# Expert groups of up to three tiles in one fixed pass, with the first layer computed already turned

## The reference

```python
scores = np.where(mask, scale * q @ k.T + bias, -1e9)       # window 128, batch 4, 8 heads, seq 576, dim 64
x = (softmax(scores) @ v).transpose(0, 2, 1, 3).reshape(2304, 512)
logits = x @ w_gate                                          # 8 experts
expert_idx = np.argmax(logits, axis=1)
gate_w = softmax(logits)[np.arange(N), expert_idx]
# each expert takes its tokens in order, up to capacity (576)
h = np.maximum(disp @ w1[e], 0.0)                            # [rows, 512] @ [512, 1024]
y = h @ w2[e]                                                # [rows, 1024] @ [1024, 512]
out[i] = gate_w[i] * y[expert_idx[i], pos[i]]
```

## Time and profile before

| what | value |
|---|---|
| median of 3 runs | 413.89 us (413.81 to 414.29) |
| profiled execution, its own time | 414.16 us |
| its span, first to last instruction | 412.5 us |
| mean granted TensorE clock | 0.993 |
| PE busy | 398.3 us (97%) |
| DVE, ACT, POOL busy | 254.8, 200.1, 146.0 us |

### The profile page before, as it was taken

One profiled execution on the slowest core, in us unless ns is written; L12 is line 12 of the kernel. 1 busy time (PEld: TensorE's weight loads), 2 busy tenths in 40 slices (PEclk: granted clock), 3 DMA queues, 4 the chain that ended last, 5 costly groups with the idle time before them and its releaser, 6 DMA issues.

```text
span 412.5 us, 10630 instructions
## 1 busy us (share of the span) xinstructions
PE 398.3 (97%) x2630; PEld 326.3 (79%) x2631; DVE 254.8 (62%) x802; ACT 200.1 (49%) x530; POOL 146.0 (35%) x228
## 2 busy tenths in 40 slices
PE   7999999999999999999999999999999999999991
PEld 7688888887877777888888888888888888888871
DVE  6787776889798578755566355526755566323220
ACT  2978778877867434555333155223555433122210
POOL 7548888725634423123221123221122221122201
PEclk9999999999999999999999999999999999999997
DMA  9999999999320115656766235706556760111100
GB/s 163 194 294 210 239 235 248 287 229 213 75 78 28 53 27 191 219 207 206 248 226 184 95 107 201 244 25 188 182 197 199 245 216 25 51 51 40 51 25 17
DMA packets 80971, 64.08 MB, mean 155 GB/s; under 512 B 63726, under 2 KB 63726, under 8 KB 80944
## 3 DMA queue, kind: packets, MB, share of 16 engines
q1 hardware_dynamic: 73600, 52.19, 46.4%
q0 software_dynamic: 3520, 10.76, 8.0%
q10 hardware_dynamic: 3824, 0.80, 1.2%
HBM read 54.29 MB, written 10.23 MB: 156 GB/s over the span
## 4 chain that ended last, share of the span: by engine, by line
PE 89%; DVE 4%; SPq 3%; DMA 1%; issue 1%; POOL 0%; ACT 0%; POOLq 0%; DVEq 0%
PE ps L1431 30%; PE ps L1463 18%; PE ps L1467 9%; PE ps L1264 7%; PE ps L1291 7%; PE ps L1451 4%; PE ps L1302 4%; PE ps L1236 4%; PE ps L1272 3%; PE ps L1424 2%; SPq L360 2%; DMA q_rows<-in_q 1%; DVE ps L871 1%; DVE probs L884 1%; PE ps L1348 0%
## 5 line engine op out<-in xcount | busy, mean ns | idle before, releaser
L1431 PE MATMUL ps<-weights_sb,rowsT_hi 128*128 (+1 forms) x336 | 107.8, 402 | 0.0
L809 ACT ACTIVATE hidden<-ps 128x512 f32<-128x512 f32 x20 | 12.0, 598 | 141.4 <-PE ps L1431 89.5
L1463 PE MATMUL ps<-weights_sb,hiddenT_hi 128*128 x320 | 79.2, 390 | 0.5 <-ACT hiddenT_hi L813 0.5
L1168 DVE TENSOR_TENSOR weights_sb<-raw,weights_sb 128x1024 f32 (+1 forms) x56 | 67.1, 1219 | 15.6 <-issue 13.3
L646 POOL DMA_INDIRECT out<-y_sb,dst_now x20 | 20.2, 1008 | 151.5 <-DVE y_sb L1175 151.5
L1431 PEld LDWEIGHTS ps<-weights_sb,rowsT_hi 128*128 128x128 f32 x336 | 61.1, 188 | 13.9 <-issue 0.6
L1463 PEld LDWEIGHTS ps<-weights_sb,hiddenT_hi 128*128 128x128 f32 x320 | 60.0, 188 | 13.3 <-issue 0.7
L1431 PE MATMUL ps<-weights_sb,rowsT_lo 128*128 (+1 forms) x168 | 66.2, 394 | 0.0
L1148 DVE TENSOR_TENSOR hiddenT_lo<-ps,hiddenT_hi 128x512 fp32r<-128x512 f32 x40 | 25.8, 686 | 57.2 <-ACT hiddenT_hi L813 57.2
L798 ACT ACTIVATE weights_sb<-raw 128x1024 f32 (+1 forms) x56 | 56.6, 1068 | 0.0
L696 ACT ACTIVATE probs<-probs,mins 128x128 f32<-128x128 f32 x144 | 55.6, 393 | 0.2 <-DVE mins L884 0.2
(11 more groups left out here) (177 smaller groups left out, 602.2 us busy)
## 6 DMA issues: line engine op xcount, KB each, us to landing
raw<-in_moe_w SPq DMA_DIRECT2D x64, 512.0 KB, 4.1
q_rows<-in_q SPq DMA_DIRECT2D x16, 256.0 KB, 6.0
v_rows<-in_v SPq DMA_DIRECT2D x16, 256.0 KB, 5.7
x_rows<-x_sb SPq DMA_DIRECT2D x16, 256.0 KB, 4.7
k_rows<-in_k SPq DMA_DIRECT2D x14, 256.0 KB, 5.9
k_rows<-in_k ACTq DMA_DIRECT2D x2, 256.0 KB, 7.2
v_rows<-in_v SPq DMA_DIRECT2D x4, 128.0 KB, 6.3
v_front<-in_v SPq DMA_DIRECT2D x4, 128.0 KB, 6.1
```

The costliest lines, as they stand in the source:

```text
L1168: vec.tensor_tensor(weights_sb[:, slot, 2 * layer + 1, part].rearrange("p s n -> p (s n)"), raw[:, j, :], weights_sb[:, slot, 2 * layer, p ...
L1431: ins = te.matmul(dst, left[a], right[c], start=first and n == 0, stop=last and n == 2)
L1463: te.matmul(y_ps(j), hiddenT[0][:, c, :], weights(slot, kind, D * c, D), start=(c == 0 and kind == 2), stop=False)
```

## The change

Experts are done one after another in a fixed pass, `group(n)` for n = 0 to 7, each with up to three tiles side by side (two for expert 0, whose first tile is done as before). The first layer now holds a 128x128 piece of the weights and moves the tiles' turned rows, 256 or 384 columns at once, so that the hidden layer comes out already turned; PE has no `turn_hidden`. The hidden features are made in eight chunks `c`; chunk c's second layer stands two steps behind its first, so a group has ten steps, and three PSUM banks and three SBUF buffers go round (`RINGED`). From expert 1 on, each step asks whether the expert has a third tile (`third`) and takes the code for three or for two. The three gathers, row transposes, weighings and scatters of a group are always done, also where the third tile is empty. Weight blocks are split in a fixed order, one per step, with addresses known beforehand. Tiles beyond the third of an expert go through a loop at the end, with their weights loaded again. Most of DVE's table arithmetic (`make_tables`) now stands behind the first chunk of group 0.

```diff
-    PAIRS = -(-MOST // 2)
-    TILES = 2 * PAIRS + 3
+    SIDE = 3
+    TABLE = -(-N // P)
+    RINGED = 3
+    TURNED_AT = (3, 4, 5)
...
-        hidden_ps = lambda half: ps[:, half, :]
-        hiddenT_ps = lambda half: ps[:, 2 + half, :]
-        rowsT_ps = ps[:, 4, :]
-        y_ps = lambda j: ps[:, 5 + j, :]
+        first_hidden_ps = lambda half: ps[:, half, :]
+        first_hiddenT_ps = lambda half: ps[:, 2 + half, :]
+        first_y_ps = ps[:, 5, :]
+        hiddenT_ps = lambda c, size: ps[:, c % RINGED, 0:P * size]
+        y_ps = lambda i: ps[:, RINGED + i, :]
+        rowsT_ps = lambda i: ps[:, 6 + i % 2, :]
...
+            def gather(n):
+
+                if not (isinstance(n, int) and n == 0):
+                    pool.wait_ge(rows_turned, tiles_before(n))
+                    pool.wait_ge(weight_kept, n)
+                if isinstance(n, int) and n > 0:
+                    rows = src_row[:, KEEPS * n:KEEPS * n + SIDE]
...
+                for i in range(sides(n)):
+                    wait_alone(pool, y_ready, tile_count(n, i))
+                    g.indirect_dma_start(out, bass.IndirectOffsetOnAxis(ap=rows[:, i:i + 1], axis=0),
+                                         y_sb[:, i, :], None, bounds_check=N - 1, oob_is_err=False
+                                         ).then_inc(scattered, 16)
...
+            gather(0)
             pool.wait_ge(first_y_ready, 1)
             g.indirect_dma_start(out, bass.IndirectOffsetOnAxis(ap=first_dst_i[:, 0:1], axis=0),
                                  first_y[:, :], None, bounds_check=N - 1, oob_is_err=False
                                  ).then_inc(first_scattered, 16)
-            pool.wait_ge(tables_ready, 1)
+            gather(1)
+            gather(2)
             pool.wait_ge(dst_ready, 1)
             pool.wait_ge(first_scattered, 16)
-            tiles = pool.value_load(tiles_to_i[0:1, E - 1:E], min_val=1, max_val=TILES)
-            with pool.Fori(0, PAIRS) as pair:
-                with pool.If(pair * 2 + 1 <= tiles):
-                    for o in (1, 2):
-                        t = pool.snap(pair * 2 + o)
-                        with pool.If(t < tiles):
-                            gather(t + 2, o % 2)
-                        with pool.If(t <= tiles):
-                            if o == 2:
-                                finish_scatter(t - 2)
-                            else:
-                                with pool.If(pair > 0):
-                                    finish_scatter(t - 2)
-                            scatter(t - 1, (o + 1) % 2)
-            pool.wait_ge(scattered, tiles * 16)
+            scatter(0)
+            for n in range(1, E):
+                if n + 2 < E:
+                    gather(n + 2)
+                finish_scatter(n - 1)
+                scatter(n)
...
+            def relu(n, c):
+                size = sides(n)
+                act.wait_ge(hidden_done, n * FC + c + 1)
+                nc.scalar.activation(hiddenT[0][c % RINGED][:, 0:P * size], hiddenT_ps(c, size),
+                                     ACT.Relu).then_inc(hiddenT_hi, 1)
+
+            def group(n):
+                for c in range(FC):
+                    relu(n, c)
+                    if n + 1 < E:
+                        split_hi(c // CHUNKS, n + 1, c % CHUNKS)
+                        if c in TURNED_AT:
+                            rows_hi(n + 1, c - TURNED_AT[0])
...
+            def lower(n, c):
+                size = sides(n)
+                dve.wait_ge(hiddenT_hi, n * FC + c + 1)
+                vec.scalar_tensor_tensor(out=hiddenT[1][c % RINGED][:, 0:P * size], in0=hiddenT_ps(c, size), scalar=0.0,
+                                         in1=hiddenT[0][c % RINGED][:, 0:P * size].bitcast(F32),
+                                         op0=ALU.max, op1=ALU.subtract).then_inc(hiddenT_ready, 1)
...
+            def weigh_all(n):
+                dve.wait_ge(weight_kept, n + 1)
+                if not (isinstance(n, int) and n == 0):
+                    dve.wait_ge(y_free, n)
+                for i in range(sides(n)):
+                    weigh(n, i)
+
+            def group(n):
+                for c in range(FC):
+                    lower(n, c)
+                    if n == 0 and c == 0:
+                        make_tables()
+                    if n + 1 < E:
+                        split_lo(c // CHUNKS, n + 1, c % CHUNKS)
+                        if c in TURNED_AT:
+                            rows_lo(n + 1, c - TURNED_AT[0])
+                        if c == TURNED_AT[-1]:
+                            keep_weights(n + 1)
+                weigh_all(n)
+
+            for i in range(SIDE - 1):
+                rows_lo(0, i)
+            keep_weights(0)
...
+            def make_tables():
+                link(vec.scalar_tensor_tensor(out=is_free[:, :], in0=is_free[:, :], scalar=float(2 * N),
+                                              in1=src_f[:, :], op0=ALU.mult, op1=ALU.add))
+                vec.tensor_copy(dst_row[:, :], is_free[:, :]).then_inc(dst_ready, 1)
+                te = [P, TABLE, E]
+                vec.tensor_scalar(extra[:, 1:E], tiles_of[:, 1:E], -float(SIDE), 0.0, ALU.add, ALU.max)
...
+            for n in range(E):
+                group(n)
...
+            def first_layer(n, size, c):
+                for d in range(DC):
+                    last = product(hiddenT_ps(c, size), [weights(parity(n), kind, F * d + P * c, P) for kind in (0, 1)],
+                                   [part[:, d, 0:P * size] for part in rowsT[parity(n)]], d == 0, d == DC - 1)
+                last.then_inc(hidden_done, 1)
+
+            def second_layer(n, size, c):
+                if c == 0:
+                    pe.wait_ge(w_split[1], n * CHUNKS + CHUNKS)
+                    if not (isinstance(n, int) and n == 0):
+                        pe.wait_ge(y_ready, tiles_before(n))
+                pe.wait_ge(hiddenT_ready, n * FC + c + 1)
+                for i in range(size):
+                    last = product(y_ps(i), [part[c % RINGED][:, P * i:P * i + P] for part in hiddenT],
+                                   [weights(parity(n), kind, D * c, D) for kind in (2, 3)], c == 0, c == FC - 1)
+                    if c == FC - 1:
+                        last.then_inc(y_done[i], 1)
+
+            def step(n, size, c):
+
+                if c < FC:
+                    first_layer(n, size, c)
+                if c >= RINGED - 1:
+                    second_layer(n, size, c - (RINGED - 1))
+
+            def rows_and_weights(n):
+                pe.wait_ge(rowsT_ready, all_count(n))
+                pe.wait_ge(w_split[0], n * CHUNKS + CHUNKS)
+
+            def group(n, third):
+                for c in range(FC + RINGED - 1):
+                    if third is None:
+                        step(n, SIDE - 1, c)
+                    else:
+                        with pe.If(third > 0):
+                            step(n, SIDE, c)
+                        with pe.If(third < 1):
+                            step(n, SIDE - 1, c)
+                            if c == FC + RINGED - 2:
+                                pe.sem_inc(y_done[SIDE - 1], 1)
+                    if c in TURNED_AT and n + 1 < E:
+                        turn_rows(n + 1, c - TURNED_AT[0])
...
-            turn_rows(0, 0, 16)
-            first_second_layer(range(FC - 2, FC)).then_inc(first_y_done, 1)
-
-
-            pe.wait_ge(rowsT_ready, 1)
-            first_layer(0, 0, slice(0, 1))
-            first_layer_chunks(1, 0, slice(0, 1), range(1))
-            turn_rows(1, 1, 16)
+            turn_rows(0, 0)
+            first_second_layer(range(FC - 2, FC - 1))
+            pe.wait_ge(filled_ready, 1)
+            turn_rows(0, 1)
+            first_second_layer(range(FC - 1, FC)).then_inc(first_y_done, 1)
+            rows_and_weights(0)
+            group(0, None)
+            pe.wait_ge(first_y_ready, 1)
+            pe.wait_ge(sizes_ready, 1)
+            for n in range(1, E):
+                third = pe.value_load(third_i[0:1, n:n + 1], min_val=0, max_val=1)
+                rows_and_weights(n)
+                group(n, third)
             pe.wait_ge(tables_ready, 1)
-            tiles = pe.value_load(tiles_to_i[0:1, E - 1:E], min_val=1, max_val=TILES)
-            first_layer_chunks(1, 0, slice(0, 1), range(1, DC)).then_inc(hidden_done, 1)
-            pe.wait_ge(first_y_ready, 1)
-            with pe.Fori(0, PAIRS) as pair:
-                for o in (1, 2):
-                    t = pe.snap(pair * 2 + o)
-                    with pe.If(t <= tiles):
-                        now, before = expert_of(t), expert_of(t - 1)
-                        pe.wait_ge(hidden_even, t)
-                        with pe.If(t < tiles):
-                            pe.wait_ge(rowsT_ready, t + 1)
-                            pe.wait_ge(w_split[0], now * CHUNKS + CHUNKS)
-                            first_layer(0, o % 2, pe.snap(now & 1))
-                        pe.wait_ge(hidden_odd, t)
```

(15 more changed lines are left out.)

453 lines of the change are left out of this document (205 added, 248 removed).

## The result

The changed kernel takes 401.99 us (median of 4 runs, 401.73 to 402.08) against 413.85 us for the kernel before on the same chip (4 runs, 413.67 to 414.29): ratio 0.9711, 95% interval [0.9694, 0.9728]. The span of the profiled execution is 400.0 us, before 412.5. The forecast was 405.5, its range 399.5 to 411.5: the sign and the reason hold, the gain was 11.9 us where 8.4 were forecast.

What follows compares the result with a forecast made beforehand. TensorE (PE) was taken as the bound. Its work from 155.63 us fell from 248.3 to 238.3 (-10.0); with stalls +0.5 and tail +1.15 that made -8.4, span 404.1, median 405.5 us, range 399.5 to 411.5.

Steps and rivals of the forecast that it cites:

- Bound and sign: Whole kernel: PE is the bound, and dropping 160 hidden-row transposes at 0.109 us saves 17.4 us, so it gets faster.
- First layer: 768 narrower matmuls instead of 480, excess paid per matmul (0.125 and 0.178 us): 116.4 us against 111.9, plus 4.5.
- the column reading: First-layer rival: excess goes with the columns, or less; 0.116 and 0.174 us a matmul give 400.5 us; chance 0.08.
- The rule on loads: First-layer rival: held-operand loads of 0.188 us run fully in series with the matmuls, 130 us more, 536; chance 0.01.
- Second layer: Same 480 matmuls of 512 columns, as products of three in a row at 0.230 us instead of 0.227: +1.6 us.
- Row transposes: Turning gathered rows: seven groups always turn three tiles, 21 after the hand-over instead of 19, at 0.44 us: +0.9.
- Hand-over: Start of group 0: both its tiles must be turned, cast and split before its first matmul: +1.3 us.
- Tables in group 0: DVE's table arithmetic, 4.0 us, delays a split and the second `lower`, stalling PE by 1.0 us.
- The unseen stalls: In the pass: an allowance for rounded stalls not seen in any row, +0.5 us.
- Tail: After PE's end: three scatters instead of one, +0.55 us, and one more register load, +0.6: together +1.15.
- Conditional steps and code: Rival in the pass: 70 conditional steps or missed code fetches cost PE time, 419.5 us at 0.2 a step; chance 0.05.
- Hand-offs that stall each group: Rival: PE stalls 0.5 us in every group, or first groups wait for the third gather: 409 to 412.8 us; chance 0.13.

Runs made afterwards that it cites:

- e1: Changed kernel with the 160 removed transposes put back as dead work that nothing reads: 419.4 us, ratio 1.0125 to the kernel before.
- e4: Changed kernel with the first layer of two-tile groups done one tile at a time, 768 matmuls of 128 columns instead of 384 of 256: 441.5 us.
- e5: Changed kernel with second-layer products reordered: per chunk all tiles with the upper part of hiddenT, then all with the lower: 402.9 us, pass 233.51.
- e8: Changed kernel with both group 0 tiles turned together, group 1's gathers issued before the first scatter, and DVE's tables in two pieces: 400.61 us.
- e3: Changed kernel with DVE's tables of group 0 in two pieces, behind chunks 1 and 6, instead of one piece behind chunk 0: 401.77 us.
- e7: Changed kernel with the last group's last two second-layer chunks run tile by tile and the register load moved ahead of the last scatters: 400.42 us.
- e2: Changed kernel without its conditions, each group's two- or three-tile code fixed for these inputs: 402.71 us, pass 233.50 against 233.52.
- e10: Changed kernel with TensorE always computing three tiles in all seven groups after group 0, without asking for the third: 434.57 us, ratio 1.0499.

## Why the prediction was right, and where its sizes were off

**Bound and sign** were right. The whole gain comes from the transposes, priced from a piece of the chain: 17.4 by forecast, 17.0 to 17.4 in e1.

**First layer**: the term that was off. I took an excess per matmul (0.125 and 0.178, 116.4 us). Measured over the pass are 0.119 and 0.1745: 45.64 + 67.02 = 112.7 us, 3.7 less. Beyond the bare columns (0.107 and 0.160) that is 0.012 and 0.0145, at 512 columns 0.014 to 0.020: it grows with the columns, though not quite in proportion, so the other reading (0.116 and 0.174, 111.4 us) came nearer. A single excess at one size cannot tell the two readings apart, and I let the nearby load pace of the earlier trace rows, 0.12 from four loads, decide for the dearer one; e4 shows that this floor, 0.112, lies just below the pace of 256 columns and leaves it alone. The trace before had one more hint, which I read for another purpose: the eight transposes of the earlier trace rows, 128 columns and a load each, are 0.109 apart, so 0.12 need not be a floor; their loads are shorter, though (0.140 us against 0.188 for those of the products). By the column reading the forecast would have been 400.5, as the rival says; the measured 402.0 lies nearer to it than to my 405.5, and I had given that rival a chance of only 0.08.

**The rule on loads.** The pass has a load of 0.188 for each matmul and a pace of 0.1175 with 256 columns; in series the two would be 0.295. Loads do not wait for the matmul ahead of them to end, and their own durations overlap. The Trainium skill ("TensorE: Matmul & The Clock Gate", Part 3, "What overlaps and what doesn't"), by which a whole-array load could not overlap the matmul in flight, is not borne out by these traces; the rival that followed from it gave 536 us.

**Second layer** +1.6: the size was right (0.2303 on average), the reason wrong, so the hit is luck. It isn't the order (e5); the slower matmuls are those behind a first-layer chunk, and the cause stays open.

**Row transposes** +0.9: 0.44 a tile and 21 of them in the pass, as forecast. The kernel before was misread: it turned 20 tiles behind the hand-over, not 19 (84 transposes in all, 80 of them from 159.2 us on), so the difference is +0.4, and its loop's entry had 1.3 us of small waits, not 1.8. The two errors cancel, since the forecast sums the new pass and sets it against the measured 248.3.

**Hand-over**: 1.3 forecast, 1.1 measured; 0.5 of it comes back when both tiles are turned together (e8).

**Tables in group 0**: 1.0 forecast, 0.97 measured, at the place and behind the instructions that were named (18 small steps ran, not the 16 counted, in the 4.0 us forecast). What I didn't see was the next one in line: group 1's first gather, behind the first scatter on GpSimd, costs 0.25 once the tables are out of the way (e3). It is gone when the gathers go first (e8).

**The unseen stalls**, +0.5: there are none. 112.7 + 110.6 + 9.2 + 1.0 = 233.5 is the whole pass, and apart from the wait on the tables no two starts are more than 0.34 us apart.

**Tail**: 1.15 forecast, 2.1 measured. I let three indirect DMAs follow each other at their own 1.0; they start 1.29 apart, the issue between them counts. The last starts 2.90 after PE's end, not 2.35 (0.55 of the gap). The register load's 0.6 is as forecast (e7). The last 0.4 is the stretch behind it, until the engines have drained, and stays unassigned.

**Rivals.** Conditional steps and code: nothing that e2 can measure. The Trainium skill ("Runtime: NRT & Kernel Launch", "Instruction fetch mechanics") has a taken branch beyond the fetched window stall; the trace shows 32 fetches instead of 13 and no stall beside them. How far any jump here reaches beyond fetched code the traces don't tell, so the rule itself is not tested. Hand-offs that stall each group: only group 0, once. Weights or GpSimd as a bound in two-tile groups: excluded by e10.

**The sum again**: by measured terms -14.8 (pass) + 1.1 + 2.1 = -11.6, and the medians differ by 11.9. Forecast -8.4. The difference of 3.5 is the first layer (-3.7) and the stalls that didn't come (-0.5), less the tail (+0.95), with a few tenths of small terms. Two terms were off in opposite directions, so the sum looks better than its parts.

## What to carry to other kernels

Where TensorE is the bound, swapping the held and the moving operand so that the result comes out already turned is worth the transposes it saves: the price is more, narrower matmuls, and down to 256 columns they cost here little more than their share of the columns (0.119 us against half of 0.233); at 128 they cost twice it (e4). Take a matmul's pace from pieces of the chain at two sizes at least, never from the mean duration or from one size. When an engine off the path has a block of small steps to do once, put it where the next thing that it owes the busy engine is furthest off, and look for who is second in line: e3 lost again a quarter of what it removed, and only with the gathers moved too came the whole. At the end of a program make the last pieces unequal: what is finished early can leave early.

## What the runs showed of the hardware

- The pace of these matmuls, each with a load of its own, at 2.4 GHz: 128 columns 0.1125 us, 256 0.1175 to 0.12, 384 0.1735 to 0.1755, 512 0.227 to 0.233. At 128 columns it is twice what the columns need, a floor of some 0.11. Transposes of 128 columns, whose loads are shorter (0.140 us against 0.188), are 0.109 apart.
- 70 conditional steps on PE and 32 instead of 13 code fetches cost no measurable time in a pass in which PE is never idle but for one wait.
- Scatters at the end of GpSimd's program start 1.29 to 1.33 us apart, though each is 0.98 long: 0.3 of issue stands between them.
- A step at the end of GpSimd's program counts in full: with one register load moved ahead of the last scatters, the stretch behind the last one's start was 0.6 us shorter.
